# A first tile with its own program: both quads in separate buffers, ScalarE writes the blocks, weights split behind it

## What is computed

```python
for t in range(S):
    cur = np.einsum('bhd,bhe->bhde', u[None] * kt, vt)
    y[:, :, t] = np.einsum('bhd,bhde->bhe', rt, state + cur)
    state = wt[:, :, :, None] * state + np.einsum('bhd,bhe->bhde', kt, vt)
```

## Time and profile before

| | |
|---|---|
| median of 3 runs | 724.79 us (723.89 to 725.16) |
| the profiled execution, its own time | 725.35 us |
| its span, first to last instruction | 723.5 us |
| PE busy / weight loads busy | 83% / 73% of the span |
| DVE / ACT / POOL busy | 70% / 44% / 31% |
| mean granted clock of TensorE | 0.958 of full speed |

### The profile page before, as it was taken

How to read it: one execution, slowest core, us unless ns; L and a number is a source line. 1 busy time by engine, 2 the same in 40 slices (tenths; PEclk the granted TensorE clock), 3 DMA queues, 4 the chain that set the end, 5 groups by cost and what they waited for, 6 DMA issues and landing times.

```text
span 723.5 us, 12474 instructions
## 1 busy us (share of the span) xinstructions
PE 603.3 (83%) x4549; PEld 527.8 (73%) x4549; DVE 508.8 (70%) x1297; ACT 320.6 (44%) x693; POOL 221.0 (31%) x193
## 2 busy tenths in 40 slices
PE   0534799979998999899989998899979899985892
PEld 0423788969887888788878888788879889972242
DVE  5793889488949794889578967987698854542413
ACT  1522344544464536453644474446534546452012
POOL 4451233244224332432242423342334223220000
PEclk9965999999999999999999999999999999996897
DMA  9941304310422041214021313112310019863336
GB/s 294 341 152 43 110 3 153 103 53 2 154 80 74 2 153 29 87 40 154 8 98 50 101 55 103 50 57 99 105 49 18 2 44 415 343 213 136 128 134 262
DMA packets 44295, 81.39 MB, mean 112 GB/s; under 512 B 4160, under 2 KB 26816, under 8 KB 44224
## 3 DMA queue, kind: packets, MB, share of 16 engines
...
...
## 4 chain that ended last, share of the span: by engine, by line
PE 58%; DVE 23%; ACT 8%; issue 6%; POOL 2%; DMA 1%; SPq 1%; DVEq 0%; ACTq 0%; POOLq 0%
PE yb L773 20%; PE hb L760 18%; DVE zs L942 4%; PE ab L686 4%; PE ab L705 3%; PE ab L711 3%; DVE ang L1090 3%; DVE r_end L978 2%; DVE ang L1098 2%; DVE A L989 2%; PE ab L724 2%; PE pb L783 2%; PE yb L887 1%; DVE tmp L956 1%; ACT turns L572 1%
## 5 line engine op out<-in xcount | busy, mean ns | idle before, releaser
L489 POOL TENSOR_TENSOR g_lo<-ang,g_hi 128x384 fp32r<-128x384 f32 x128 | 129.4, 1011 | 403.0 <-DVE g_hi L1103 403.0
L760 PE MATMUL hb<-x_hi,win 128*128 128x384 f32 x768 | 219.5, 340 | 26.3 <-DVE ang L1098 19.6
L773 PE MATMUL yb<-wout,g_hi 128*128 128x384 f32 x768 | 206.1, 349 | 2.4 <-POOL g_lo L489 2.4
L760 PEld LDWEIGHTS hb<-x_hi,win 128*128 128x128 f32 x768 | 141.6, 189 | 33.8 <-DVE ang L1098 26.6
L773 PEld LDWEIGHTS yb<-wout,g_hi 128*128 128x128 f32 x768 | 133.3, 189 | 14.1 <-issue 7.2
L578 ACT ACTIVATE ang<-ang 128x384 f32<-128x384 f32 x128 | 67.2, 525 | 164.7 <-DVE ang L1090 164.6
L773 PE MATMUL yb<-wout,g_lo 128*128 128x384 f32 x384 | 129.2, 336 | 0.0
L760 PE MATMUL hb<-x_lo,win 128*128 128x384 f32 x384 | 129.1, 336 | 0.0
L572 ACT ACTIVATE turns<-hb 128x384 int32<-128x384 f32 x128 | 62.8, 491 | 117.4 <-PE hb L760 117.4
L1090 DVE SCALAR_TENSOR_TENSOR ang<-turns,hb 128x384 f32<-128x384 int32 x128 | 70.6, 552 | 61.9 <-ACT turns L572 61.2
L1098 DVE SCALAR_TENSOR_TENSOR ang<-ang,hb 128x384 f32<-128x384 f32 x128 | 69.8, 546 | 46.6 <-ACT ang L580 46.6
...
## 6 DMA issues: line engine op xcount, KB each, us to landing
...
```

The source lines that it names most:

```text
L489: g.tensor_tensor(g_lo[f % RING][:, :], ang[f % 2][:, :], g_hi[f % RING][:, :].bitcast(F32), ALU.subtract).then_inc(glo_done, 1)
L760: last = t.matmul(hb[f % 2][:, 0:TT], win[:, f, w, k, :], x[:, k, :], start=(n == 0), stop=(n == 3 * DK - 1))
L773: last = t.matmul(yb[c][:, 0:DM], gx[f % RING][:, c * P:(c + 1) * P], wout[:, f, w, :], start=(f == 0 and n == 0), stop=(f == NF - 1 and n ...
```

## The change

The first tile gets a program of its own, `first_tile()` on each engine, and `tile_steps` begins with tile 0 as `mid`.
- Quad 1 has second buffers (`k_end1`, `r_end1`, `seed1`, `k_end_tok1`, `A1`, `r_tok1`, `k_tok1`, `diag1`, `ptot1`, `flags1`), which lie where `x_hi` and its neighbours lie later, and each quad has four PSUM banks of its own (`FIRST_BANKS`). `yT` and `scaled` stay single.
- ACT writes the twelve diagonal blocks of each quad (`first_diagonal`), not DVE. The carried state is zero in the first tile, so chunk 0 has no `scaled` and no matmul for it.
- SP loads both quads ahead of all weights; the weights come as w_in, w_out, w_in, ... (`WEIGHT_ORDER`), `phi` last.
- ACT's split of parts 0 to 3 stands inside and behind the first tile, that of 4 to 7 in slots 1, 3, 5, 7 of the second layer of tile 0. The low parts: DVE makes 0 and 1 behind its first tile, POOL 2 and 3; POOL makes 4 and 5 in slots 2 and 5, DVE 6 and 7 in slots 6 and 8 of tile 0's second layer. PE waits for each low part where it first uses it (`low_part`).
- Counts of semaphores move by one tile; later tiles keep their instructions.

```diff
-ACT_PARTS = {0: [0], 3: [1, 2, 3], 6: [4, 5], 7: [6, 7]}
-POOL_PARTS = {0: [0], 5: [2], 8: [6]}
-DVE_PARTS = {3: [1], 9: [3, 4], 13: [5, 7]}
+WEIGHT_ORDER = [n + half * NSTAGE for n in range(NSTAGE) for half in range(2)]
+ACT_PARTS = {1: [4], 3: [5], 5: [6], 7: [7]}
+POOL_FIRST, POOL_PARTS = [2, 3], {2: [4], 5: [5]}
+DVE_FIRST, DVE_PARTS = [0, 1], {6: [6], 8: [7]}
+LOW_BY_POOL = POOL_FIRST + [n for slot in sorted(POOL_PARTS) for n in POOL_PARTS[slot]]
+LOW_BY_DVE = DVE_FIRST + [n for slot in sorted(DVE_PARTS) for n in DVE_PARTS[slot]]
...
+        FIRST_BANKS = [[ab[0], ab[1], yb[0], pb], [hb[0], hb[1], yb[1], yb[2]]]
...
-            load_quad(0, 0)
-            load_tokens(0, 0)
-            sp.dma_start(ub[:, :], u_d).then_inc(small_in, 16)
-            sp.dma_start(phi[:, :, :], phi_d.rearrange("(k p) n -> p k n", p=P)).then_inc(small_in, 16)
-            for i in range(2 * NSTAGE):
+            def load_first(q):
+                for dst, src in ((zs[q], zs_d), (zp[q], zp_d)):
+                    sp.dma_start(dst[:, :], src[0, q]).then_inc(decay_in[q], 16)
+                sp.dma_start(kT[q][:, :], kt_d[0, q]).then_inc(first_k_in[q], 16)
+                if q == 0:
+                    sp.dma_start(ub[:, :], u_d).then_inc(u_in, 16)
+                sp.dma_start(FIRST_RTOK[q][:, :, :, :], rtok_d[0, q]).then_inc(first_rk_in[q], 16)
+                sp.dma_start(FIRST_KTOK[q][:, :, :, :], ktok_d[0, q]).then_inc(first_rk_in[q], 16)
+                sp.dma_start(rT[q][:, :], rt_d[0, q]).then_inc(first_r_in[q], 16)
+                sp.dma_start(v_tok[q][:, :, :, :], vtok_d[0, q]).then_inc(v_in[q], 16)
+            for q in range(QUADS):
+                load_first(q)
+            for i in WEIGHT_ORDER:
...
+            def first_tile():
+                for q in range(QUADS):
+                    wait_apart(pool, (suffix_done, 0, QUADS, q + 1))
+                    pool.wait_ge(first_k_in[q], 16)
+                    g.tensor_tensor(FIRST_K_END[q][:, :], kT[q][:, :], zs[q][:, :], ALU.mult).then_inc(k_end_done, 1)
+                    if q == 0:
+                        pool.wait_ge(u_in, 16)
+                    pool.wait_ge(first_rk_in[q], 32)
+                    reading_product(0, q, FIRST_RTOK[q], FIRST_KTOK[q])
+                for n in POOL_FIRST:
+                    low_of_weights(n)
...
+            def first_diagonal(q, cs):
+                act.wait_ge(diag_done, q + 1)
+                for c in cs:
+                    for h in range(4):
+                        a.activation(FIRST_A[q][:, h % 2, c, h // 2, :], ident[:, :], ACT.Copy,
+                                     scale=FIRST_DIAG[q][:, c, h:h + 1]).then_inc(first_blocks[q], 1)
...
+            def first_y(q):
+                if q:
+                    act.wait_ge(x_in[0], XQ)
+                for pp in range(PAIRS):
+                    act.wait_ge(first_full[q], Y_MADE - PAIRS + pp + 1)
+                    a.copy(yT[0:DD, pp, :], FIRST_BANKS[q][2 + pp][0:DD, 0:TT]).then_inc(first_y_read[q], 1)
...
+            def first_tile():
+                act.wait_ge(consts, NCONST)
+                first_keys(0)
+                first_diagonal(0, (0, 1))
+                first_keys(1)
+                first_diagonal(0, (2,))
+                first_states(0)
+                high_of_weights(0)
+                first_diagonal(1, (0, 1, 2))
+                first_y(0)
+                first_states(1)
+                high_of_weights(1)
+                high_of_weights(2)
+                first_y(1)
+                high_of_weights(3)
...
-                    if first:
-                        for i in ACT_PARTS.get(slot, []):
-                            hi_of_weights(i)
+                    if mid == 0:
+                        for n in ACT_PARTS.get(slot, []):
+                            high_of_weights(n)
...
+            def first_tile():
+                first_keys(0)
+                first_products(0, (0, 1), FIRST_BANKS[0][2:4])
+                first_sums(0)
+                first_flag(0)
+                first_products(0, (2,), FIRST_BANKS[0][0:2])
+                first_keys(1)
+                first_sums(1)
+                first_products(1, (0, 1), FIRST_BANKS[1][2:4])
+                first_flag(1)
+                first_products(1, (2,), FIRST_BANKS[1][0:2])
+                first_y(0)
+                first_y(1)
...
+                    if T == 0 and f % (NF // NSTAGE) == 0:
+                        low_part(2 * f // (NF // NSTAGE))
...
+            def first_settle(q):
+                dve.wait_ge(first_full[q], A2_DONE)
+                v.tensor_reduce(vsum[:, :], FIRST_BANKS[q][1][0:1, 510:512], X, ALU.add).then_inc(chain, nth(own))
+                chained()
+                v.tensor_copy(verdict[q][:, :], vsum[:, :]).then_inc(verdict_done, 1)
+                dve.wait_ge(first_state[q], CH)
+                chained()
+                general_path(0, q, FIRST_BANKS[q], FIRST_A[q], FIRST_DIAG[q], FIRST_SEED[q])
+                dve.sem_inc(a_done, 1)
+            def first_tile():
+                for q in range(QUADS):
+                    decays(0, q, FIRST_PTOT[q])
+                    chained()
+                    scale(0, q, FIRST_PTOT[q], FIRST_SEED[q])
+                    if q:
+                        diagonal_sum(0, 0, FIRST_RTOK[0], FIRST_DIAG[0])
+                    prefix(q, FIRST_SEED[q], FIRST_R_END[q])
+                    reading(0, q, FIRST_R_END[q])
+                    bounds(q, FIRST_FLAGS[q])
+                diagonal_sum(0, 1, FIRST_RTOK[1], FIRST_DIAG[1])
+                for q in range(QUADS):
+                    first_states(q)
+                    first_triangle(q, (0, 1), FIRST_BANKS[q][2:4], A01_DONE[q]).then_inc(first_a_read[q], 1)
+                    first_triangle(q, (2,), FIRST_BANKS[q][0:2], A2_DONE).then_inc(chain, nth(own))
+                    first_settle(q)
+                for n in DVE_FIRST:
+                    low_of_weights(n)
+                make_fold()
...
+                    if mid == 0:
+                        for n in DVE_PARTS.get(slot, []):
+                            low_of_weights(n)```

On **DVE**, at the start of the program (names are those of the buffers, their numbers left out), the order before was, for quad 0:

```order
L947 TENSOR_SCALAR fine<-ptot 128x6
L949 TENSOR_REDUCE wmax<-zp 128x1
L956 TENSOR_TENSOR tmp<-ptot,fine 128x6
L967 TENSOR_REDUCE diag<-r_tok 128x12
L971 TENSOR_REDUCE vsum<-ab 1x1
L978 SCALAR_TENSOR_TENSOR r_end<-zp,seed 128x768
L989 TENSOR_SCALAR A<-ident,diag 128x128 x4
L982 TENSOR_TENSOR r_end<-rT,r_end 128x768
L984 CAST verdict<-vsum 1x1
L989 TENSOR_SCALAR A<-ident,diag 128x128 x8
L1162 TENSOR_TENSOR win<-win_raw,win 128x4x384
L997 COPY_PREDICATED A<-mask,ab 128x512 x2
```

More of the change, by code:

```diff
@@ L243, in build @@
         w2 = [[w2_homes[g][j][:, :].rearrange("p (f n) -> p f n", n=DM) for j in range(4)] for g in range(2)]
+        FIRST_K_END, FIRST_R_END, FIRST_SEED = [k_end, k_end1], [r_end, r_end1], [seed, seed1]
+        FIRST_K_TOK, FIRST_A, FIRST_DIAG, FIRST_PTOT = [k_end_tok, k_end_tok1], [A, A1], [diag, diag1], [ptot, ptot1]
+        FIRST_FLAGS = [flags, flags1]
+        FIRST_RTOK, FIRST_KTOK = [r_tok, r_tok1], [k_tok, k_tok1]
         hb = [ps(f"hb{i}") for i in range(2)]
@@ L929, in nth, with chained, decays @@
                 return 1
-            def attention(T, q, step, own):
+            def chained():
+                dve.wait_ge(chain, own[0])
+            def decays(T, q, total):
+                wait(dve, decay_in[q], T, 32, 32)
+                v.tensor_reduce(wmax[:, 1:2], zs[q][:, P - 2::P], X, ALU.max, apply_absolute_value=True).then_inc(chain, nth(own))
+                chained()
+                for m in range(CHUNKS):
+                    part = zs[q][:, m * P:(m + 1) * P][:, ::-1]
+                    last = v.tensor_tensor_scan(part, part, ends[:, ::-1], 0.0, ALU.mult, ALU.add)
+                last.then_inc(suffix_done, 1)
+                wait(dve, suffix_done, T, QUADS, q + 1)
+                v.tensor_tensor(total[:, :], zp[q][:, 1::P], zs[q][:, ::P], ALU.mult).then_inc(chain, nth(own))
+                chained()
+                v.tensor_scalar(fine[:, :], total[:, :], P_LEAST, None, ALU.is_ge).then_inc(chain, nth(own))
@@ new lines, in bounds @@
+            def bounds(q, out):
+                v.tensor_reduce(wmax[:, 0:1], zp[q][:, :], X, ALU.max, apply_absolute_value=True).then_inc(chain, nth(own))
+                chained()
+                v.tensor_reduce(wmax1[:, :], wmax[:, :], X, ALU.max).then_inc(chain, nth(own))
+                chained()
+                v.tensor_scalar(out[:, 1:2], wmax1[:, :], 1.0, None, ALU.is_le).then_inc(chain, nth(own))
+                chained()
+                v.tensor_reduce(out[:, 0:1], fine[:, :], X, ALU.add).then_inc(flag_done, 1)
@@ L935, in attention @@
-                    wait(dve, decay_in[q], T, 32, 32)
```

(30 more changed lines are left out.)

364 lines of the change are left out of this document (232 added, 132 removed).

## The result

| | before | after |
|---|---|---|
| median of 4 runs | 724.83 us (723.89 to 725.16) | 714.09 us (713.25 to 715.53) |
| ratio, 95% interval | | 0.9856 [0.9838, 0.9874] |
| profiled execution / its span | 725.35 / 723.5 us | 714.17 / 712.4 us |
| PE / weight loads busy | 83% / 73% | 85% / 74% |
| DVE / ACT / POOL busy | 70% / 44% / 31% | 71% / 46% / 32% |

A forecast was written before the change was run, and what follows sets the result against it. PE and DVE were taken to bound the kernel by turns from tile 0's second layer on. 725.35 us less 20.8 (earlier `x_hi`) plus 7.3 (second layer) gave 711.85, as a median 711.3, rounded to 711.5; range 701 to 719.

The forecast's parts named there:

- Step 1: Start of tile 0: the new order of loads costs nothing, each load being ahead of its use.
- Step 2: First tile, both quads: POOL blocks DVE for some 8.4 us; `diag` of quad 1 ends at 30.2 us.
- Rival 1: First tile and weight parts: DVE is hardly blocked, POOL waits instead; 696 to 705 us, chance 0.22.
- Step 3: First tile to its outputs: ACT's diagonal blocks take 0.31 us each, both copies `yT` are out at 38.4 us.
- Step 4: SP's queue after `yT`: quad 1's small DMAs follow tile 1's loads; `x_hi` at 50.3 us, 20.8 us earlier.
- Step 5: Tile 0's second layer: late weight parts sum to 10.3 us, 3.02 fall into DVE's free time, 7.3 added.
- Rival 2: Additions cost all they are, ACT's blocks take 0.48 us, a split delays `yT`; 717 to 722 us, chance 0.14.
- Rivals 3 and 4: 3: tile 0's clock stays low, slower, chance 0.03. 4: wait moves into SP's queue or weights, no change, chance 0.02.

The follow-up runs named there:

- products_dve: Kernel after, but DVE itself makes both products of each quad in the first tile, POOL only `k_end`: 712.73 us.
- pool_none: Kernel after, but POOL makes no weight parts; DVE makes low parts 0 to 5 ahead of tile 0's second layer, ACT high parts 1 to 5 likewise: 711.02 us.
- staggered2: Kernel after, but DVE finishes quad 0 right after quad 1's decays; weights re-placed, POOL's two parts early, DVE's last three in slots 5, 10, 12: 699.52 us.
- dve_blocks: Kernel after, but DVE in place of ACT writes the first tile's diagonal blocks, ahead of each quad's states: 715.64 us.
- hold_q1: Kernel after, but SP issues tile 1's loads for quad 1 only when quad 1's five small DMAs have landed: 714.81 us.
- xraw_first: Kernel after, but SP issues quad 1's five small DMAs of tile 0 ahead of tile 1's seven loads for quad 0: 712.27 us.
- shadow: Kernel after, but all eight weight splits are made ahead of tile 0's second layer, all low parts by DVE: 706.14 us.
- dve_late: Kernel after, but DVE's two low weight parts move from slots 6 and 8 to slots 10 and 12: 712.38 us.
- before_again: The kernel before, without an edit, run for a second trace: 725.08 us.
- both_moves: Kernel after, with quad 1's small DMAs ahead of tile 1's loads and weights out of slots 1 to 9 except ACT's in 1 and 3: 703.48 us.

## Why the prediction was nearly right, step by step

**Step 1, the loads cost nothing:** held. DVE starts its scans at 5.05 us, after 1.00 us of waiting for `zp` (1.78 in the kernel before), and quad 1's at 16.34, behind no DMA. (The slices of DMA sum to 5.55 MB at 18.8 us, not 5.51; nothing hangs on it.)

**Step 2, DVE and POOL in both quads:** held, 7.7 us blocked for 8.4; quad 1's `diag` ends at 28.85 for 30.2. Rival 1, that POOL would wait instead, fell with products_dve and pool_none. The rule of the Trainium skill that the prediction weighed ("SBUF — State Buffer", section "Who interferes with whom") is that the later of the two blocks: the timeline agrees where POOL's row began first (7.24 and 7.29 us, and 9.25 and 9.38). Where POOL came second, it paid too: its weight row at 72.47 began 0.67 us behind a DVE product with two inputs (71.80), and took 4.20 us for the 3.45 of staggered2. And `g_lo`, which PE needs, took 2.44 us beside DVE's weight row of 95.95, for 1.01 elsewhere. POOL lost less by this than DVE did where it came second.

**Step 3, to the outputs:** held. A block is 0.30 us for 0.31; `yT` of quad 0 is out at 36.65 for 38.4, earlier because step 2 was, and because two pieces overlap that the sum had in a row. Part of that is this execution's luck: the six other kernels with the same code up to there have it out at 37.4 to 37.9. With dve_blocks the ACT blocks are seen to be worth 2.2 to 2.6 us.

**Step 4, SP's tail:** the mechanism held and the size failed. From `yT` to `x_hi` it was to be 11.9 us and was 16.6. The term that was too small is what comes behind the loads: I had taken the time from before's start of the sequence to its quiet DMAs, and 0.3 us for the small DMAs' own bytes, with nothing for the landing, though the row of before had 2.25 us for one on quiet DMAs. hold_q1 shows what the sequence takes, 15.5 us from the first issue to `x_hi`: the full stretch ends 13.0 us after the first issue, not 11.5, for it holds part of their 288 KB too (at 342 GB/s, the stretch's mean, all of it would be 0.9 us); then 1.5 us of the thin end and 1.0 to `x_hi`. The kernel after needs 1.0 us more than that; the other kernels with loads behind need 0.2 to 0.9 more, so these loads may be the reason, but that isn't shown. xraw_first takes the backlog away and gets 4.5 us back. Of the 4.7 us, 1.75 were made good by step 3's early end: 2.9 net.

**Step 5, tile 0's second layer:** the mechanism held, and the term was too small: 9.5 for 7.3. With shadow's 0.8 explained by its late `x_lo`, the late parts cost the whole 9.5 of the 10.3 that the sum charged: the term that failed is the free time, 0.8 us of it used where the sum took off 3.02. Taken away one source at a time, DVE's two give 3.1 back (dve_late) and POOL's two 5.0 (pool_none, with two of ACT's splits), 8.1 together; alone, each costs more than that, for what is left then stands 6.4 us (POOL's) and 4.5 us (DVE's) over before. So the two overlap, and the 9.5 can't be divided between them cleanly. ACT's four splits were not tested apart. The lower granted clock in these stretches is not shown to cost anything by itself: in the second and third (0.86 and 0.93) it goes with PE's waits and is at 1.00 in shadow, and in the first it was 0.88, and 0.90 in before_again, whose distance is 70.3. Its own share of the 9.5 is not known.

**Rival 2**, that the additions cost all they are, was nearly true in its first half (9.5 of 10.3), but not in its second, for ACT's blocks were at 0.30. **Rivals 3 and 4** fell: the distance grew by 9.5 and not by the 20 that a low clock for six slots would take, and `x_hi` came at 53.2, not after 63.

**What no step had:** 2.8 us at the end of the program. 1.0 lies in the routing and expert stages, whose instructions are the same. The windows from `x_hi` of tile 7 to the end, of the kernel before and then of the kernel after:

```profile
582.00:723.50 141.50, 112.56 (x758) 83.50 (x752) 55.90 (x129) 49.60 (x104) 20.78 (x23) 0.89 0.59 214
```

```profile
574.00:712.40 138.40, 111.27 (x754) 82.96 (x752) 55.89 (x129) 49.36 (x104) 20.53 (x22) 0.91 0.60 219
```

DVE's busy time is the same to 0.01 us, PE's is 1.3 us less at a granted clock of 0.91 for 0.89. I read that as luck, and the other traces speak for it: from `x_hi` of tile 7 to DVE's last instruction both traces of before have 121.1 and 121.4 us, nine of the kernels with the new first tile 119.9 to 120.3, but two of them, hold_q1 and both_moves, 121.5 and 121.2. That the clock makes the difference is a reading of these windows, not shown. The 1.8 us are the end of the stores, below. Without these two the profiled execution would stand at 717.0, and not 2.3 but 5.1 us over the sum: the prediction's nearness is in part their doing.
